# Attention and two feed-forward stages on one core: VectorE's order of work in the first pair of heads

## What is computed

```python
scores = scale * np.matmul(q, k.transpose(0, 1, 3, 2))       # B, H, S, D = 4, 8, 576, 64
scores = np.where(causal, -1e9, scores)
a = np.exp(scores - scores.max(-1, keepdims=True))
a /= a.sum(-1, keepdims=True) + 1e-09
local = np.matmul(a, v)
q_p = phi(q)                                                 # exp(min(x, 0)) + max(x, 0)
mem_ret = np.einsum('bhsd,bhde->bhse', q_p, M_prev)
mem_norm = np.einsum('bhsd,bhd->bhs', q_p, z_prev)[..., None] + 1e-6
g = 1.0 / (1.0 + np.exp(-beta))[None, :, None, None]
attn = g * mem_ret / mem_norm + (1 - g) * local
...
x = (silu(x @ w_gate) * (x @ w_val)) @ w_out                 # 2304 x 512, width 1536
...                                                          # second stage: width 2048, another activation
```

## Time and profile before

| what | value |
|---|---|
| runs of the kernel before, us | 991.40, 988.88, 989.84; median 989.84 |
| profiled execution, whole time | 990.56 us |
| its span, from first to last instruction | 988.7 us |
| TensorE busy | 965.2 us (98%) |
| VectorE busy | 709.6 us (72%) |
| ScalarE busy | 463.1 us (47%) |
| GpSimd busy | 309.8 us (31%) |

### The profile page before, as it was taken

The page is one execution under the profiler, slowest core; times in us unless marked ns, Lnnn a source line. Parts: engine busy times, 40 slices in busy tenths (PEclk is TensorE's granted clock), DMA queues, the critical chain, the costliest instruction groups (busy, mean ns, idle before and its releaser), DMA issues.

```text
span 988.7 us, 18774 instructions
## 1 busy us (share of the span) xinstructions
PE 965.2 (98%) x6328; PEld 921.2 (93%) x6328; DVE 709.6 (72%) x1370; ACT 463.1 (47%) x938; POOL 309.8 (31%) x291
## 2 busy tenths in 40 slices
PE   6999999999999999999999999999999999999998
PEld 4777777889999999999999999999989999999998
DVE  5888999567787555457555479788896777866666
ACT  5899999555444222233232254545543334423331
POOL 5677776186672200002000056475350000000000
PEclk9999999999999999999999999999999999999999
DMA  6544543389888756555555533767774835548321
GB/s 234 165 154 163 159 155 109 121 298 347 310 283 321 237 217 222 207 192 192 198 217 220 223 139 128 254 226 272 275 270 167 298 148 204 190 162 294 134 111 65
DMA packets 46156, 204.72 MB, mean 207 GB/s; under 512 B 5488, under 2 KB 5872, under 8 KB 46064
## 3 DMA queue, kind: packets, MB, share of 16 engines
q1 hardware_dynamic: 45920, 203.52, 57.2%
q10 hardware_dynamic: 144, 0.00, 0.0%
HBM read 147.33 MB, written 56.17 MB: 206 GB/s over the span
## 4 chain that ended last, share of the span: by engine, by line
PE 84%; ACT 5%; issue 4%; DVE 4%; DMA 2%; POOL 1%; ACTq 0%; DVEq 0%; SPq 0%; POOLq 0%
PE ps L1416 24%; PE ps L1417 24%; PE ps L1418 24%; PE ps L1391 5%; PE ps L1334 4%; ACT pt L800 3%; PE ps L1364 3%; DMA kept_ul<-wu_l 1%; DVE xt_l L1091 1%; DVE xy L1207 1%; ACT rown L779 1%; DMA betas<-beta 1%; DVE hid_l L1185 1%; ACT tmp L905 0%; DMA wu_r<-w_up 0%
## 5 line engine op out<-in xcount | busy, mean ns | idle before, releaser
L1416 PE MATMUL ps<-xt_h,wu_h 128*128 128x384 f32 x840 | 281.6, 335 | 3.5 <-ACT u2s L875 1.6
L1418 PE MATMUL ps<-xt_h,wu_l 128*128 128x384 f32 x840 | 280.7, 334 | 0.0
L1417 PE MATMUL ps<-xt_l,wu_h 128*128 128x384 f32 x840 | 280.7, 334 | 0.0
L1416 PE MATMUL ps<-hid_h,wd_h 128*128 128x384 f32 x672 | 225.7, 336 | 5.0 <-DVE xy L1207 4.9
L1418 PE MATMUL ps<-hid_h,wd_l 128*128 128x384 f32 x672 | 224.6, 334 | 0.0
L1417 PE MATMUL ps<-hid_l,wd_h 128*128 128x384 f32 x672 | 224.6, 334 | 0.0
L1207 DVE TENSOR_TENSOR xy<-xy,ps 128x384 f32<-128x384 f32 x288 | 158.2, 549 | 68.4 <-PE ps L1418 67.5
L890 ACT ACTIVATE hid_h<-hid_r 128x768 fp32r<-128x768 f32 x84 | 70.8, 842 | 205.5 <-DVE hid_r L1181 143.2
L1416 PEld LDWEIGHTS ps<-xt_h,wu_h 128*128 128x128 f32 x840 | 157.7, 188 | 6.5 <-issue 3.4
L1417 PEld LDWEIGHTS ps<-xt_l,wu_h 128*128 128x128 f32 x840 | 157.7, 188 | 0.0
L1418 PEld LDWEIGHTS ps<-xt_h,wu_l 128*128 128x128 f32 x840 | 157.7, 188 | 0.0
(11 more groups left out here) (84 smaller groups left out, 1267.7 us busy)
## 6 DMA issues: line engine op xcount, KB each, us to landing
wu_l<-kept_ul SPq DMA_DIRECT2D x40, 896.0 KB, 8.6
wu_h<-kept_uh SPq DMA_DIRECT2D x40, 896.0 KB, 6.9
kept_uh<-wu_h SPq DMA_DIRECT2D x20, 896.0 KB, 7.2
kept_ul<-wu_l SPq DMA_DIRECT2D x20, 896.0 KB, 9.0
wd_h<-kept_dh SPq DMA_DIRECT2D x28, 512.0 KB, 3.6
wd_l<-kept_dl SPq DMA_DIRECT2D x28, 512.0 KB, 4.6
wu_r<-w_up SPq DMA_DIRECT2D x20, 512.0 KB, 5.5
qk<-qk_in SPq DMA_DIRECT2D x15, 640.0 KB, 5.0
```

What stands on the lines that cost most here:

```text
L1416: nc.tensor.matmul(dst, w_hi, v_hi, start=start, stop=False, skip_group_check=onto)
L1417: nc.tensor.matmul(dst, w_hi, v_lo, start=False, stop=False, skip_group_check=onto)
L1418: return nc.tensor.matmul(dst, w_lo, v_hi, start=False, stop=stop, skip_group_check=onto)
```

## The change

On VectorE, for the first pair only, the order of instructions is another. The maxima of tile 0 are taken ahead of the local shares; the reciprocal for the shares stands between these maxima and `qp`; the maxima of tile 1 and then the two copies into `cf` stand ahead of the norms. No instruction is added or removed, and the other engines' lists are the same.

```diff
-            nc.vector.memset(cf[0:D, :, 0], 1.0).then_inc(cf_set, 1)
+            dve.wait_ge(maskf_set, 2)
+            tile_max(0)
+            nc.vector.memset(cf[0:D, :, 0], 1.0).then_inc(cf_set, 1)
             nc.vector.reciprocal(gone[:], gexp[:, 1]).then_inc(gone_set, 1)
+            phi(0)
+            tile_max(1)
             dve.wait_ge(gone_set, 1)
             rest = gone[:].rearrange("p (h o) -> p h o", o=1)
             nc.vector.tensor_copy(cf[:, :, 1:NT], rest.broadcast_to([P, 2 * NPAIR, NT - 1])).then_inc(cf_set, 1)
             nc.vector.tensor_copy(cf[D:P, :, 0], gone[D:P]).then_inc(cf_set, 1)
-            dve.wait_ge(maskf_set, 2)
-            tile_max(0)
-            phi(0)
             for p in range(NPAIR + 2):
...
                 if p < NPAIR:
                     mem_scale(j)
                     for k in range(1, SLOTS):
-                        tile_max(j + k)
+                        if p > 0 or k > 1:
+                            tile_max(j + k)
                     mem_scale(j + 1)
```

## The result

| | median, us | lowest to highest | runs |
|---|---|---|---|
| kernel before | 990.23 | 988.82 to 992.61 | 22 |
| changed kernel | 992.18 | 990.26 to 995.17 | 22 |

The ratio is 1.0024, with a 95% interval of 1.0018 to 1.0030. The forecast was 991.2 us, the range 988.9 to 993.4, with 0.84 for "no change beyond 0.3%". The profiled execution took 992.39 us, its span is 990.5 us.

What follows compares the result with a forecast made beforehand. TensorE was taken as the bound, busy 965.2 of 988.7 us. Norms 2.0 us late shrink to 1.15 at VectorE's copy and 1.0 at the end; known executions average 990.2, forecast 991.2 us, range 988.9 to 993.4.

Steps and rivals of the forecast that it cites:

- Step 1: On VectorE, tile 0's maxima go ahead of the shares: gain between 0 and 0.15 us, taken as 0.1.
- Steps 2 to 4: VectorE's norms, behind tile 1's maxima and the shares' copies, and TensorE's first eight transposes: both 2.0 us later.
- step 2: On VectorE, memset and reciprocal ahead of `qp` make it and GpSimd's products 0.4 us later, costing nothing by itself.
- Step 5: On VectorE, tile 2's maxima start at 15.41 instead of 14.50, 0.91 us later; pair 1's scores may start at 17.16.
- Steps 6 to 8: From VectorE's copy of the second transposes to the first block's scores: 0.85 to 1.15 us late, taken as 1.0.
- step 8: First block's scores: 0.85 us late if VectorE's last `mscale` precedes GpSimd's next products, 1.15 if GpSimd is first; taken 1.0.
- step 6: VectorE's copy of the second transposes waits for all eight: 1.15 us later, as are the last transposes (20.00 becomes 21.15).
- step 7: On ScalarE, tile 1's exponentials start earlier, at 12.86 instead of 14.07, but tile 3's 0.5 us late; not deciding.
- the clock comes later: Rival, chance 0.35: TensorE stays at half pace behind the longer pause; 1.85 to 3.5 us late, 992.1 to 993.7 us.
- the case to which I had given 0.50: Main forecast, chance 0.50: VectorE's new order in the first pair makes the end 0.85 to 1.15 us late.
- Nothing reaches the path: Rival, chance 0.11: unseen slack in tile 2's and pair 1's work leaves 0 to 0.5 us delay, 990.2 to 990.7.
- faster: Rival, chance 0.04: tile 1's earlier exponentials shorten pair 1, by 0.85 us at most, to 989.4 us.

Runs made afterwards that it cites:

- e1: Changed kernel plus ten unread 128x128 matmuls on TensorE between tile 3's scores and the first eight transposes; ratio 1.0016, pair 2 1.00 us later than before.
- e8: Changed kernel plus unread matmuls in all early TensorE pauses (nine at the start, five behind tile 0's scores, seven behind tile 3's); ratio 0.9993.
- e6: Changed kernel plus nine unread 128x128 matmuls on TensorE before the first input is there; ratio 1.0003, pair 2 1.08 us later than before.
- third profile: Changed kernel, nothing altered, profiled a third time; pair 2 starts 1.70 us later than in the kernel before.
- second profile of the changed kernel: Changed kernel, nothing altered, profiled once more; pair 2 starts 3.10 us later than in the kernel before.

## Why the prediction was right, and where it was not

- **Step 1** (0 to 0.15 us gained, taken 0.1): 0.00 measured. The shares had been hidden completely, also because the scores run at half pace.
- **Steps 2 to 4** (norms and first transposes 2.0 us late): 2.14 and 2.13 late against the first scores (14.22 - 5.76 - 6.32, and 16.39 - 5.76 - 8.50). The mechanism and the size were right; only `qp`, 0.4 late in step 2, came 0.28 late, and it didn't decide.
- **Step 5** (tile 2's maxima 0.91 late): 15.74 - 5.76 is 9.98 instead of 8.87, 1.1 late.
- **Steps 6 to 8** (0.85 to 1.15 us at the end, taken 1.0): 1.00 in e1, where the pace was up by the transposes, as the steps had assumed. That the number is met so well is in part luck. VectorE came ahead of GpSimd's product there and its last `mscale` took 0.16 us, the case for which step 8 had 0.85. The copy of step 6 was 1.42 us late instead of 1.15 and the last transposes 1.30; the wait of 0.30 us ahead of the first block's scores went away, and these were 0.84 late; then TensorE waited 0.15 us for the values that GpSimd scales, a wait that no step had. In step 7 tile 3's exponentials were to be 0.5 us late; in the changed kernel, at half pace, they were 0.92.
- **What failed is the weight of the cases.** The steps had the first transposes at full pace, since those of the kernel before had reached it while they ran, and "the clock comes later" got 0.35. It came later in all three profiled executions of the changed kernel, and in two of them it is the larger part of the loss: 0.7, 1.6 and 2.1 us on top of the 1.0 that e1 shows for the order. The rival's own size, 1.85 to 3.5 us, held 2.61 and 3.10 and just missed 1.70, because in that execution the scores behind the transposes had the full pace for a part. I had weighed "4 us of matmuls still stand ahead of the pause, as before". In the profile of before these had not been enough either: the pace doubled only during the transposes behind them.
- The measured 992.18 is inside the range, but the range reached that far up for this rival's sake: it lies at the rival's lower edge (992.1 to 993.7) and 1 us above my forecast, and the loss is about twice the 1.0 us of the case to which I had given 0.50. A median over executions that lose 1.7 to 3.1 us at pair 2 can't be laid on one mechanism; what the profiles show is that both act.
- **Nothing reaches the path** and **faster** are out for this kernel. "Faster" has its truth in e8: with TensorE's clock up, tile 1's maxima do fit in the wait.
- The Trainium skill, TensorE: Matmul & The Clock Gate, says in "What's actually happening" that activity releases the throttle; e1, e6 and e8 agree. By its Part 4, that transposes don't count as such activity, I had put the end at the later side of the rival's 1.85 to 3.5 us. One profile of three came out there, at 3.10. Whether transposes count stays open: in the third profile the pace doubled behind 1.86 us of transposes, while scores ran, and in the kernel before it doubled during transposes, behind 3.57 us of scores. No kernel here ran transposes alone.
- The Trainium skill's rule on the ports that VectorE and GpSimd share (SBUF — State Buffer, "Who interferes with whom") held in both orders: 0.16 us when VectorE came first, 0.96 to 1.17 when GpSimd's product had begun, and then both ended together.

## What to carry to other kernels

Before work is moved into an engine's wait, ask when its input will be there, not how long the wait is: here VectorE stood idle from 10.3 to 11.95, but tile 1's scores came at 12.2, so the work pushed the critical norms instead of filling the gap. Count a new pause on TensorE twice, once for its length and once for the matmuls behind it, which may run at half pace. And an order of work should be judged at the clock at which it will run: the same one lost 1 us at one level and won 1 us at the other.

## What the runs showed of the hardware beyond that

- The clock does not only come late, it falls again. In e6 it was up from 6.5 to 9.5 us, and down to 0.50 from about 10 to 20 us, behind a stretch in which TensorE was busy 1.26 of 3 us.
- The granted clock of a stretch can't be trusted at the start of a trace: in the changed kernel it reads 1.00 while eight matmuls take 2.40 us instead of 1.30.
- There is a second such place, at 215 to 225 us, where TensorE waits for ScalarE and GpSimd. TensorE waits there in kernels with and without filling, and in some executions the clock falls. The table of windows for e1 shows the clock at 0.83 there, and 36 matmuls:

```profile
215.00:225.00 10.00, 8.09 (x36) 7.47 (x35) 5.37 (x8) 5.00 (x9) 8.27 (x8) 0.83 0.81 289
```

  The changed kernel's profiled execution ran 49 in the same 10 us, with the clock at 1.00:

```profile
215.00:225.00 10.00, 8.68 (x49) 8.06 (x48) 7.66 (x10) 6.22 (x11) 8.72 (x9) 1.00 0.81 293
```

  The second profile of the changed kernel shows 0.83 and 36 as well, and took 995.1 us. A clock of 0.83 over 10 us takes 1.7 us of work at full pace away (10 x 0.17), an estimate. Over a whole execution the two with this dip have a clock of 0.998. By that sign it is the more frequent one in the changed kernel: 9 of its 22 executions have 0.998, and of the 98 executions of the kernel before that were made beside the experiments, at other times, 9 have. It makes the longest executions (994.4 to 995.2 us) but not the loss: the 13 executions at 1.00 have the same median, 992.18, as all 22. I did not try to remove it, and why a change in the first 20 us should favour it stays open.
